# One spread moved from VectorE to ScalarE, roundings an iteration later, gate columns by transposes, three more zero products

## The reference

```python
for t in range(S):                                  # attention, per batch and head
    m_new = np.maximum(f_gate[:, :, t] + m, i_gate[:, :, t])
    f_stab = np.exp(f_gate[:, :, t] + m - m_new)
    i_stab = np.exp(i_gate[:, :, t] - m_new)
    C = f_stab * C + i_stab * outer(vt, kt)
    n = f_stab * n + i_stab * kt
    y[:, :, t] = sigmoid(o_gate[:, :, t]) * (C @ qt) / max(abs(n . qt), 1)
h = x @ w_in; P = a0 + a1*h + a2*h**2 + a3*h**3     # first feed-forward block
Q = 1 + abs(b0)*abs(h) + abs(b1)*h**2
x = (P / (Q + 1e-6)) @ w_out
xn = x / rms(x) * rms_g                             # second feed-forward block
out = (silu(xn @ w_gate) * (xn @ w_val)) @ w_out
```

## Time and profile before

| | |
|---|---|
| time, median of 3 runs | 471.13 us (468.38 to 481.77) |
| profiled execution: its time | 468.82 us |
| profiled execution: its span | 467.0 us |
| granted TensorE clock, mean | 1.000 |
| PE, DVE, ACT, POOL busy | 98%, 70%, 62%, 54% |
| attention | about the first 72 us of the span |
| transition, attention and first block interleaved | about 72 to 113 us |
| the two feed-forward blocks | to the end |

### The profile page before, as it was taken

One profiled execution on the slowest core, in us unless ns is written; L12 is line 12 of the kernel. 1 busy time (PEld: TensorE's weight loads), 2 busy tenths in 40 slices (PEclk: granted clock), 3 DMA queues, 4 the chain that ended last, 5 costly groups with the idle time before them and its releaser, 6 DMA issues.

```text
span 467.0 us, 7429 instructions
## 1 busy us (share of the span) xinstructions
PE 455.5 (98%) x2679; PEld 398.8 (85%) x2680; DVE 328.5 (70%) x462; ACT 289.4 (62%) x468; POOL 250.6 (54%) x271
## 2 busy tenths in 40 slices
PE   8999999988999999999999999999999999999997
PEld 4888997866999888998899888888888888888886
DVE  7999997998899998999999543484343444534333
ACT  6788887799889999999988648532111222211111
POOL 4476698858898897988989555981000000000000
PEclk9999999999999999999999999999999999999999
DMA  8998930230000000000005030000010000100001
GB/s 245 332 317 267 268 92 1 91 135 1 0 1 1 1 1 1 0 1 0 2 0 214 2 135 3 0 1 0 1 56 1 0 0 1 44 14 1 1 0 58
DMA packets 8372, 26.78 MB, mean 57 GB/s; under 512 B 1216, under 2 KB 3136, under 8 KB 7824
## 3 DMA queue, kind: packets, MB, share of 16 engines
q1 hardware_dynamic: 8336, 26.30, 17.6%
HBM read 24.33 MB, written 1.97 MB: 56 GB/s over the span
## 4 chain that ended last, share of the span: by engine, by line
PE 82%; DVE 5%; ACT 3%; issue 2%; POOL 1%; DVEq 0%; POOLq 0%; ACTq 0%
PE ps L1620 7%; PE ps L1621 7%; PE ps L1622 7%; PE ps L1550 6%; PE ps L1552 6%; PE ps L1551 6%; PE ps L1568 4%; PE ps L1569 4%; PE ps L1570 4%; PE ps L1528 4%; PE ps L1526 4%; PE ps L1527 4%; PE ps L1624 3%; PE ps L1625 3%; PE ps L1474 2%; PE ps L1529 2%
## 5 line engine op out<-in xcount | busy, mean ns | idle before, releaser
L992 ACT ACTIVATE ab<-ps 128x512 f32<-128x512 f32 x36 | 21.6, 599 | 117.6 <-PE ps L1625 117.6
L1337 DVE TENSOR_TENSOR ab<-ps,ab 128x512 f32<-128x512 f32 x36 | 24.9, 691 | 84.7 <-ACT ab L992 84.7
L589 POOL TENSOR_TENSOR qq<-qq,ab 128x512 f32<-128x512 f32 x48 | 61.2, 1296 | 20.9 <-ACT qq L836 20.8
L595 POOL TENSOR_TENSOR g_lo<-cc,g_hi 128x512 fp32r<-128x512 f32 x48 | 61.9, 1310 | 6.0 <-ACT g_hi L858 6.0
L1550 PE MATMUL ps<-wo_hi,g_hi 128*128 128x320 f32 x192 | 59.9, 312 | 2.1 <-POOL g_lo L595 1.1
L1552 PE MATMUL ps<-wo_hi,g_lo 128*128 128x320 f32 x192 | 59.3, 309 | 0.0
L1551 PE MATMUL ps<-wo_lo,g_hi 128*128 128x320 f32 x192 | 59.3, 309 | 0.0
L1568 PE MATMUL ps<-wo_hi,g_hi 128*128 128x320 f32 x136 | 42.0, 309 | 0.2 <-ACT g_hi L1000 0.2
L1570 PE MATMUL ps<-wo_hi,g_lo 128*128 128x320 f32 x136 | 42.0, 309 | 0.0
L1569 PE MATMUL ps<-wo_lo,g_hi 128*128 128x320 f32 x136 | 42.0, 309 | 0.0
L1550 PEld LDWEIGHTS ps<-wo_hi,g_hi 128*128 128x128 f32 x192 | 36.0, 188 | 5.7 <-issue 2.6
(11 more groups left out here) (189 smaller groups left out, 1252.5 us busy)
## 6 DMA issues: line engine op xcount, KB each, us to landing
qk<-q_k_dram SPq DMA_DIRECT2D x12, 448.0 KB, 9.0
wo_raw<-w_out_dram SPq DMA_DIRECT2D x7, 640.0 KB, 7.0
kv<-kv_n_dram SPq DMA_DIRECT2D x10, 372.0 KB, 6.9
w_raw<-w_main_dram SPq DMA_DIRECT2D x4, 512.0 KB, 7.7
out_dram<-y_out SPq DMA_DIRECT2D x12, 160.0 KB, 1.9
w2c_raw<-w_main_dram SPq DMA_DIRECT2D x1, 1536.0 KB, 6.2
sig_o<-o_n_dram SPq DMA_DIRECT2D x1, 1280.0 KB, 7.7
rest_raw<-w_rest_dram SPq DMA_DIRECT2D x2, 512.0 KB, 7.6
```

The source lines that it names most:

```text
L589: pool.tensor_tensor(qq[m % 2][:, h, :], qq[m % 2][:, h, :], ab[m % 2][:, h, :], ALU.mult)\
L595: pool.tensor_tensor(glo(n), cc[n // 2 % CR][:, n % 2, :], ghi(n).bitcast(F32), ALU.subtract)\
```

## The change

- ACT also spreads iteration 5, in its iteration 3, between `weights(4)` and the second sigmoid. DVE's `spread_whole(5)` is gone, and `log_weights(5)` waits for ACT's semaphore.
- `round_rest1(0)` and `round_out1(0)` go from ACT's iteration 4 to 5, and `round_out1(1)` from 5 to 6. On POOL `split_rest1(0)` goes from 5 to 6 and `low_out1(1)` from 6 to 7; on DVE `split_out1(0)` goes from 6 to 7.
- `gate_columns` uses the transpose of PE instead of a product with the unit matrix.
- Two zero products of 512 columns stand ahead of `intra(1)` and one ahead of `intra(2)`, behind its waits. All earlier ones stay.

```diff
--- before.py
+++ after.py
@@ -40,7 +40,6 @@
 COLS = (slice(1, 2), slice(2, NC))
 FIRST_O = 4
 EARLY = (7, 8, 9, 10, 11, 17, 18, 19, 20, 21, 22, 24)
-ON_DVE = 5
 WARM = 14
 ORDER = (0, 2, 4, 6, 1, 3, 5, 7)
 LAG1, LAG2 = 7, 2
@@ -646,12 +645,11 @@
                     split_main1(0)
                 elif it == 4:
                     split_main1(1)
-                elif it == 5:
+                elif it == 6:
                     split_rest1(0)
-                elif it == 6:
                     split_main1(2)
+                elif it == 7:
                     low_out1(1)
-                elif it == 7:
                     split_main1(3)
                     split_rest1(1)
                 elif it == 8:
@@ -884,7 +882,7 @@
                 weights(it + 1)
                 if it == 2:
                     gate_rows_b(1)
-                if it < NT - B and it + 2 != ON_DVE:
+                if it < NT - B:
                     spread(it + 2)
                 if it == 1:
                     gate_rows_a(1)
@@ -896,14 +894,13 @@
                     round_main1(0)
                 elif it == 2:
                     round_main1(1)
-                elif it == 4:
+                elif it == 5:
+                    round_main1(2)
                     round_rest1(0)
                     round_out1(0)
-                elif it == 5:
-                    round_main1(2)
-                    round_out1(1)
                 elif it == 6:
                     round_main1(3)
+                    round_out1(1)
                     round_rest1(1)
                 elif it == 7:
                     round_out1(2)
@@ -1251,8 +1248,6 @@
                 if it + 1 < NT - B:
                     weigh(it + 1)
                 probs(it + 1)
-                if it + 2 == ON_DVE:
-                    spread_whole(ON_DVE)
                 if it == 0:
                     gate_steps(1)
                 if it == NT - 3:
@@ -1268,7 +1263,7 @@
                     chunk_ends(1)
                 if it >= 3:
                     lo_of_x(it - 3)
-                if it == 6:
+                if it == 7:
                     split_out1(0)
                 if it == 8:
                     coefficients()
@@ -1400,8 +1395,7 @@
                     pe.wait_ge(cols_exp, 2 * i)
                 for n, c in enumerate(range(part.start, part.stop)):
                     at_ = KT * P + n * BH
-                    mm = pe.matmul(ps[:, 7, at_:at_ + BH], cumA[:, c * L:(c + 1) * L], ident[0:BH, 0:BH],
-                                   start=True, stop=True)
+                    mm = pe.transpose(ps[:, 7, at_:at_ + BH], cumA[:, c * L:(c + 1) * L], ident[0:BH, 0:BH])
                 mm.then_inc(cols_ps, 1)
 
             def gate_ends(i):
@@ -1437,10 +1431,8 @@
                 c, b = divmod(it, B)
                 if it < B:
                     pe.wait_ge(whole_spread, it + 1)
-                elif it == ON_DVE:
-                    pe.wait_ge(whole_spread, B + 1)
                 else:
-                    pe.wait_ge(spread_done, it - B + (it < ON_DVE))
+                    pe.wait_ge(spread_done, it - B + 1)
                 pe.wait_ge(low_a_done, segment(c) + 1)
                 pe.wait_ge(low_b_done, segment(c) + 1)
                 for e in range(2):
@@ -1470,6 +1462,8 @@
                     pe.wait_ge(hu_done, it)
                 else:
                     pe.wait_ge(exp_done, 2)
+                if it == 2:
+                    warm_up(1, 5)
                 for h in range(H):
                     mm = pe.matmul(psO[:, h, :], E[it % 2][:, h, :], v1[r][:, h, :], start=True, stop=True)
                 mm.then_inc(intra_done, 1)
@@ -1654,6 +1648,8 @@
                 scores(it + 1)
                 if it >= 3:
                     transposes(it - 3)
+                if it == 1:
+                    warm_up(2, 6)
                 intra(it)
                 updates(it)
             causal(NT - 1)
```

## The result

| | before | changed |
|---|---|---|
| median | 471.9 us | 475.77 us |
| lowest to highest, 10 executions each | 468.38 to 481.77 | 473.57 to 481.55 |
| ratio of the times, 95% interval | | 1.010 (1.006 to 1.014) |
| profiled execution: time, span | 468.82, 467.0 | 475.36, 473.6 |
| its mean granted clock | 1.000 | 0.986 |

The change makes the kernel about 1% slower. That is inside the 2% band, but outside the range of 467.7 to 474.0: the prediction of 470.0 was wrong.

The account below looks back on a forecast made before the run. PE was taken to bound the kernel, with DVE right behind in the attention. From 468.8 us, +0.54 for the moved wait and +0.7 for the splits gave 470.0 us; the 8-in-10 range was 467.7 to 474.0.

Parts of the forecast that it names:

- the sum: Whole kernel: 468.8 us of the profiled execution, +0.54 for the moved wait, +0.7 for the splits, giving 470.0 us.
- By this the sum stays 470.0: Clock step: rows grant 1.00 throughout from 41 us on, so the clock adds nothing to the forecast.
- the late POOL: POOL's lag of 1.5 us stays until the first feed-forward block's denominators; +0.7 us taken, bounds nothing to about 2.0.
- The base of the sum: Profiled execution before the change, 468.8 us; the median of the three runs shown, 471.13, is 0.5% above it.
- The wait moves from `sel` to `x_lo`: Ahead of transposes(1): the 0.97 us spread wait goes, 1.75 us for x_lo replaces it; net +0.54 us. Forecast chance 0.64.
- The walk along ACT's rows: ACT's chain from the exponential at 29.52 through spread, sigmoid and table loads: hi_of_x(0) ends at 38.22 instead of 36.00.
- Gate columns and zero products: PE before 24.4 us: four transposes save 0.46 us (bounds 0.2 to 0.46); the zero product ahead of intra(2) costs 0.22.
- The splits on POOL: Iterations 6 and 7: POOL's splits stretch DVE's steps and delay decay(8) to 65.7; +0.7 us taken.
- The clock: Rival, chance 0.19: the clock falls to 1.2 GHz in PE's new 1.75 us gap; +2.0, so 472.0 us.
- the long case: Clock rival with a fall twice as long: +4.0, so 474.0 us; 0.04 of its chance is beyond 2%.
- The rule against the change: Gate columns: by the skill's rule the four transposes ahead of 24.4 us count less for the clock than products; no size.
- the lower level: Clock at the start: zero products 0.43 us apart read as 1.2 GHz, four in 1.04 at 7.25 as 2.4 GHz.

Follow-up runs that it names:

- the filled versions: The changed kernel with eight zero products ahead of transposes(1), once with POOL's order as changed (473.48 us), once with low_out1(1) behind the two other splits (470.49 us).
- the filled version: The changed kernel with eight zero products of 512 columns ahead of transposes(1), where PE waits: 473.48 us, ratio 1.004 to the kernel before.
- POOL mended: The changed kernel with low_out1(1) moved behind split_main1(3) and split_rest1(1) in POOL's iteration 7: 473.14 us, ratio 1.003 to the kernel before.
- the filled version with POOL mended: The changed kernel with eight zero products ahead of transposes(1) and low_out1(1) behind the two other POOL splits: 470.49 us, ratio 0.998 to the kernel before.

## Why the prediction was wrong, point by point

Two steps of the sum failed. It put the clock at nothing ("By this the sum stays 470.0"), and it took 0.7 us for the late POOL, where the filled versions show 2.05. An estimate of an execution without a fall, from the measured terms, is 468.8 + 0.21 + 2.05 = 471.1 us, 1.1 above the sum; the filled version had 471.57 at a clock of 1.000. The rest, up to the median of 475.77, comes from the clock and from the tail: 2.2 and 2.1 us in the first trace, 4.1 us and nothing in the second (3.2 for its first fall; 0.87 for its second, 6.27 in place of 5.40).

**The base of the sum.** The sum started from the profiled execution of before, 468.8 us. That one had no fall. The executions of before have a median of 471.9, and by their mean clocks most of them have one: 21 of 29 were at 0.994 or less. The prediction saw that its base lay 0.5% below the median and set the difference aside as scatter: 3.1 of the 5.8 us that it missed stand in the median of before already. The spread from 468.38 to 481.77 was there to be read as falls of the clock in before itself.

**The wait moves from `sel` to `x_lo`.** Right. The forecast was 1.75 us at 38.99; it is 1.91 at 38.66. ACT and DVE in the changed kernel:

```profile
28.98 1.02 ACT L810 ACTIVATE E<-ps 128x1024 f32<-128x1024 f32 x1 [1.73 <-PE ps L1440]
30.03 2.44 ACT L736 ACTIVATE sel<-gA,sel 64x128 fp32r<-64x128 f32 x8
...
37.44 0.49 ACT L769 ACTIVATE x_hi<-ps 128x384 fp32r<-128x384 f32 x1
```

```profile
37.96 0.56 DVE L1193 TENSOR_TENSOR x_lo<-ps,x_hi 128x384 fp32r<-128x384 f32 x1 [1.94 <-ACT x_hi L769]
```

The walk along ACT's rows gave 38.22 for the end of `hi_of_x(0)`, and it ends at 37.93 (37.44 + 0.49). The net was +0.21 against +0.54. Nearly all of the 0.33 is that ACT's exponential starts 0.54 us earlier than before (28.98 against 29.52), not 0.24.

**Gate columns and zero products.** Four transposes from 23.44 to 23.71 take 0.27 us in place of 0.92: 0.65 saved, not 0.46. The upper bound was taken as half of the products' time, since the nearest rows were products; such a transpose takes 0.07 us here, and one of the two passes of the product 0.115. The zero product ahead of `intra(2)` costs 0.22, as forecast. The two ahead of `intra(1)` start it 0.11 later, of which nothing is left at 23.44.

**The splits on POOL.** The direction was right and the size wrong: 0.7 was taken, with 2.0 as the upper bound. The comparison of the two filled versions shows 2.05 up to the feed-forward block. The failed step is the queue: the text counted `split_rest1(1)`, `ones` and `decay(8)` behind the waiting `low_out1(1)`, and left out `split_main1(3)`, which stands there too. POOL after:

```profile
63.49 1.54 POOL L621 TENSOR_TENSOR wo_lo<-wo_raw,wo_hi 128x640 fp32r<-128x640 f32 x1 [3.69 <-DVE wo_lo L1188]
65.11 1.41 POOL L517 TENSOR_TENSOR w_lo<-w_raw,w_hi 128x512 fp32r<-128x512 f32 x1
66.60 1.29 POOL L525 TENSOR_TENSOR w_st<-rest_raw,w_st 64x512 fp32r<-64x512 f32 x1
...
68.14 0.73 POOL L511 TENSOR_TENSOR C<-C,dec 104x328 f32<-104x328 f32 x1
```

POOL stands idle for 3.69 us, and then three splits in a row push `decay(8)` to 68.14, where 65.7 was forecast. Of these 2.44 us, 1.5 are the forgotten split, 0.9 the later start, which is itself in part the first fall of the clock. The step is also wrong in what it thought late next. DVE, after:

```profile
69.01 0.67 DVE L1170 TENSOR_TENSOR C<-ps,C 40x164 f32<-40x164 f32 x2 [0.64 <-POOL C L511]
69.71 0.56 DVE L1193 TENSOR_TENSOR x_lo<-ps,x_hi 128x384 fp32r<-128x384 f32 x1
```

`state` waits for `decay`, and `lo_of_x`, which is behind `state` on DVE though it needs nothing of it, waits too. That is PE's second wait.

**The clock.** It was a rival at 0.19, and all ten executions had a mean clock of 0.989 or less. Its condition (a wait longer than any of before) was met, and its price (+2.0 for one fall, +4.0 for one twice as long) was near: the first fall cost 1.58 us in one trace and 3.2 in the other, the second 0.66 and 0.87 on top of what POOL's delay costs without any fall. Added to a base without falls it gave 472.0, and 474.0 as the long case. The reason against it was that gaps of 0.5 and 0.97 us had left the clock at 1.00. They did so in one execution; other executions of the same kernel had falls. One trace does not show how often a clock falls. The rival also took one place, while the changed kernel has falls in two.

**The rule against the change.** Nothing shows the transposes of the gate columns to lower the clock: with products in their place, the median was 483.46 us against 475.77, and the ratio to before 1.010 in both. The Trainium skill says, in "TensorE: Matmul & The Clock Gate", Part 4 (PE-mode transpose), that transposes do not count as activity for the clock as products do; no run here shows it for these four.

**What is shown and what stays open.** Shown: with the late chain of ACT left in place, keeping PE busy there and mending POOL's order brings the clocks back to 0.992 and above, and the ratio to before from 1.010 to 0.998. Shown too: the queue behind `low_out1(1)` makes the waits near 70 and 76. Supported by the traces: all eight that have a wait of 1.9 to 2.2 us in the attention have a fall that starts between 37 and 45 us, from within the wait to 2.3 us behind its end (two traces of the changed kernel, one each of six variants). Not shown: that the wait of 0.8 us near 70 brings the second fall, since four of six traces with it have none. Open: what brings the second fall; why some falls begin near 26 us behind no wait of PE at all, in an execution of the filled version and in the one with only the spread moved; and why a fall lasts 3 us in one execution and 31 in another. What the edits change is how often a fall comes and how many there are. Whether the order of ACT moves the early fall as well was not told apart.

## What to carry to other kernels

A wait that moves from one engine's result to another's is priced by its length and by what the clock does behind it. Where the times of a kernel spread by 3% and one execution shows no fall, read the mean clock of every execution before taking one as the base. When an instruction is moved past others in a queue, write out everything that stands behind it while it waits; and if PE must wait, zero products in that place can cost less than what the clock loses behind the wait (473.48 us against 475.77 here, and 470.49 against 473.14 with POOL mended).

## What the runs showed of the hardware

- In the attention and the transition the granted clock went from 1.00 to 0.50 in 13 of the 16 profiled executions. It fell in or behind all eight waits of PE of 1.9 to 2.2 us. It fell behind one of 1.28, one of 0.74, one of 0.61 and two of 0.8 us, and stayed at 1.00 behind 0.97 and 1.20 us (the two traces of before), four of 0.75 to 0.79 and four of 1.4 to 1.6 us. Twice it fell near 26 us behind no wait. A fall lasted 3.4, 6.8, 10, 20, 27 or 31 us, with PE busy for 0.96 to 1.00 of that time. In the large products none came: behind 80 us no slice of any page but the last is below 0.9.
- In the first 5 us the rate of the zero products and the listed clock don't agree. Weight loads of the changed kernel, and its window there:

```profile
3.28 0.15 PEld L1383 LDWEIGHTS ps<-warm 128*128 128x128 bf16 x1 [0.28 <-issue]
3.70 0.15 PEld L1383 LDWEIGHTS ps<-warm 128*128 128x128 bf16 x1 [0.28 <-issue]
```

```profile
3.00:4.00 1.00, 1.00 (x4) 0.30 (x3) 0.52 (x1) 1.00 (x2) 0.81 (x2) 1.00 0.74 251
```

  They are 0.42 us apart, where the product behind the zero product of 25.11 starts 0.22 later, and the window lists 1.00. The prediction read the earlier trace rows as the lower level by the rate alone; the listed clock does not bear it out, and no run tells which of the two is right.
- A transpose of 16 by 128 fp32 takes 0.07 us (four in 0.27), and the same as a product 0.23 (four in 0.92).
- The tail from the last product to the end of the span, the same instructions in every kernel, was 3.44 to 3.52 us in 13 profiled executions and 5.37 to 5.52 in three. A mean clock of 0.998 can be such a tail alone, as in the filled version with POOL mended.
